# Loading q and k as two halves, and the order of Pool's work within a head, in an attention and MLP kernel

## The reference, cut to what matters

```python
batch, n_heads, seq, head_dim = (2, 8, 768, 64)
n_clusters = 16
...
q_assign = np.argmax(np.einsum('bhsd,hcd->bhsc', q_n, c_n), axis=-1)
k_assign = np.argmax(np.einsum('bhsd,hcd->bhsc', k_n, c_n), axis=-1)
mask = q_assign[:, :, :, None] == k_assign[:, :, None, :]
scores = scale * np.matmul(q, k.transpose(0, 1, 3, 2))
scores = np.where(mask, scores, -1000000000.0)
...
return np.matmul(attn, v).astype(np.float32)
```

## Time and profile before

| what | us |
| --- | --- |
| median of 3 runs | 767.41 |
| lowest and highest | 765.59, 771.37 |
| time of the profiled execution | 765.31 |
| its span, first to last instruction | 763.5 |

### The profile page before, as it was taken

How to read it: one execution, slowest core, us unless ns; L and a number is a source line. 1 busy time by engine, 2 the same in 40 slices (tenths; PEclk the granted TensorE clock), 3 DMA queues, 4 the chain that set the end, 5 groups by cost and what they waited for, 6 DMA issues and landing times.

```text
span 763.5 us, 10199 instructions
## 1 busy us (share of the span) xinstructions
PE 711.2 (93%) x3867; PEld 631.7 (83%) x3867; DVE 398.6 (52%) x698; ACT 290.7 (38%) x604; POOL 283.9 (37%) x304
## 2 busy tenths in 40 slices
PE   4899899799998979989999999999999989899998
PEld 4788899789898978977888888888888879888886
DVE  3678888588979866585211321113111169885310
ACT  2377677566767756121010210102101055443320
POOL 3456646666645663407870000000023224740000
PEclk9999999899999999999999999999999999999999
DMA  4434423342334420203330000001031231000011
GB/s 143 130 92 112 124 73 75 99 127 54 95 90 124 120 48 1 63 28 97 110 97 1 0 1 1 0 1 56 0 111 56 50 102 42 28 14 28 28 42 55
DMA packets 26865, 48.09 MB, mean 63 GB/s; under 512 B 4032, under 2 KB 11456, under 8 KB 26560
## 3 DMA queue, kind: packets, MB, share of 16 engines
q1 hardware_dynamic: 24368, 39.49, 18.3%
q0 software_dynamic: 2448, 7.95, 3.3%
HBM read 36.41 MB, written 3.15 MB: 52 GB/s over the span
## 4 chain that ended last, share of the span: by engine, by line
PE 67%; DVE 13%; POOL 8%; ACT 4%; issue 3%; DMA 3%; SPq 2%; POOLq 0%; ACTq 0%; DVEq 0%
PE ps L1236 19%; PE ps L1352 17%; PE ps L1428 9%; PE ps L1414 6%; PE ps L1163 4%; PE ps L1149 4%; PE ps L1106 3%; DVE pt_l L807 2%; DVE row_min L800 2%; PE ps L1137 2%; DMA raw_qk<-in_k 2%; DVE mask_n L841 2%; PE ps L1138 2%; SPq L361 1%; ACT pt_h L636 1%
## 5 line engine op out<-in xcount | busy, mean ns | idle before, releaser
L1001 DVE SCALAR_TENSOR_TENSOR hid_l<-ps,hid_h 128x512 fp32r<-128x512 f32 x48 | 33.1, 690 | 203.6 <-ACT hid_h L708 203.6
L807 DVE TENSOR_TENSOR pt_l<-ps,pt_h 128x384 fp32r<-128x384 f32 x192 | 101.2, 549 | 43.1 <-ACT pt_h L636 42.3
L708 ACT ACTIVATE hid_h<-ps 128x512 fp32r<-128x512 f32 x48 | 28.7, 598 | 227.0 <-PE ps L1236 227.0
L636 ACT ACTIVATE pt_h<-ps 128x384 fp32r<-128x384 f32 x192 | 84.7, 490 | 76.6 <-PE ps L1149 75.7
L1149 PE MATMUL ps<-cst,prob 128*128 128x128 f32 x576 | 85.4, 285 | 15.1 <-ACT prob L624 9.4
L800 DVE TENSOR_REDUCE row_min<-ps 128x1 f32<-128x768 f32 x96 | 90.1, 939 | 18.0 <-PE ps L1138 17.9
L624 ACT ACTIVATE prob<-ps,row_min 128x768 f32<-128x768 f32 x96 | 87.0, 907 | 8.2 <-DVE row_min L800 7.9
L1149 PEld LDWEIGHTS ps<-cst,prob 128*128 128x128 f32 x576 | 67.2, 147 | 26.9 <-ACT prob L624 18.7
L1137 PE MATMUL ps<-k,q 80*128 80x384 f32 x192 | 75.8, 395 | 8.8 <-issue 8.0
L1352 PE MATMUL ps<-w_h,hid_h 128*128 128x512 f32 x192 | 76.1, 396 | 1.4 <-DVE x L956 1.4
L1352 PE MATMUL ps<-w_h,hid_l 128*128 128x512 f32 x192 | 75.5, 393 | 0.0
(11 more groups left out here) (158 smaller groups left out, 1607.8 us busy)
## 6 DMA issues: line engine op xcount, KB each, us to landing
w_raw<-in_moe_w_ch SPq DMA_DIRECT2D x24, 256.0 KB, 2.6
raw_d<-in_q SPq DMA_DIRECT2D x8, 384.0 KB, 3.4
raw_d<-in_k SPq DMA_DIRECT2D x8, 384.0 KB, 4.6
raw_qk<-in_q SPq DMA_DIRECT2D x16, 192.0 KB, 3.2
raw_qk<-in_k SPq DMA_DIRECT2D x16, 192.0 KB, 3.4
raw_v<-in_v SPq DMA_DIRECT2D x16, 192.0 KB, 2.5
q<-q SPq DMA_DIRECT2D x16, 192.0 KB, 2.7
k<-k SPq DMA_DIRECT2D x16, 192.0 KB, 2.7
```

The lines of the kernel that those rows point to most:

```text
L636: nc.scalar.activation(pt_h[a][:, R * hf:R * hf + R, (t % R) * P:(t % R + 1) * P], ps[:, 4 + hf, 0:HALF].rearrange("p (j c) -> p j c", j=R ...
L807: nc.vector.tensor_tensor(pt_l[a][part], ps[:, 4 + hf, 0:HALF].rearrange("p (j c) -> p j c", j=R), as_f32(pt_h[a][part]), ALU.subtract).th ...
```

## The change

The load of raw q and that of raw k get semaphores of their own. SyncE issues the load of the next q as soon as q is split, ahead of the copy of k and of the mask rows; the load of k keeps its place. Pool's `scale_q` waits for q alone, and the high part of k for k. Pool's order within a head was: split q and k, scale the next q, split w1, split v, fold. It becomes: split q and k, fold, scale the next q, split w1, split v.

```diff
             def serve(i, s, loads=True):
...
                 sp.dma_start(as_f32(q2[s][0:D, :]), as_f32(q1[s][0:D, :])).then_inc(q2_copied[s], 16)
+                if loads:
+                    sp.wait_ge(q_split, n + 1)
+                    load_q(ahead, 1 - s)
                 sp.wait_ge(k_high, n + 1)
                 sp.dma_start(as_f32(k2[s][0:D, :]), as_f32(k1[s][D:2 * D, :])).then_inc(k2_copied[s], 16)
...
                 if loads:
-                    sp.wait_ge(q_split, n + 1)
                     sp.wait_ge(k_split, n + 1)
-                    load_qk(ahead, 1 - s)
+                    load_k(ahead, 1 - s)
...
             def scale_q(n):
 
-                pool.wait_ge(qk_loaded, 32 * n + 32)
+                pool.wait_ge(q_loaded, 16 * n + 16)
...
                 if n == 0:
                     return
+                pool.wait_ge(k_loaded, 16 * n + 16)
                 high(k1[s][D:P, :], raw_qk[D:P, :]).then_inc(k_high, 1)
...
             for n in range(1, NH):
                 split_qk(n, n % 2)
+                if n >= 5 and (n - 5) % 4 < 2:
+                    fold_block((n - 5) % 4, (n - 5) // 4)
                 if n < NH - 1:
                     scale_q(n + 1)
                 if n < W1_EARLY:
                     split_w1(n)
                 split_v(n, n % 2)
-                if n >= 5 and (n - 5) % 4 < 2:
-                    fold_block((n - 5) % 4, (n - 5) // 4)
```

More of the change, by code:

```diff
@@ L178, in build @@
         cst_loaded, cen_loaded = sem("cst_loaded"), sem("cen_loaded")
-        qk_loaded, v_loaded = sem("qk_loaded"), sem("v_loaded")
+        q_loaded, k_loaded, v_loaded = sem("q_loaded"), sem("k_loaded"), sem("v_loaded")
         q2_copied = [sem(f"q2_copied{s}") for s in range(2)]
@@ L337, in _, with load_q, load_k @@
             sp.dma_start(cen[:, 0, :], centroids.rearrange("h c d -> (h c) d")).then_inc(cen_loaded, 16)
-            def load_qk(i, s):
-                for j, t in enumerate((q_t, k_t)):
-                    sp.dma_start(raw_qk[j * D:(j + 1) * D, :], t[s, i, :, :]).then_inc(qk_loaded, 16)
+            def load_q(i, s):
+                sp.dma_start(raw_qk[0:D, :], q_t[s, i, :, :]).then_inc(q_loaded, 16)
+            def load_k(i, s):
+                sp.dma_start(raw_qk[D:2 * D, :], k_t[s, i, :, :]).then_inc(k_loaded, 16)
             def load_v(i, s):
@@ L385, in _ @@
             sp.dma_start(cst[:, :], constants).then_inc(cst_loaded, 16)
-            load_qk(0, 0)
+            load_q(0, 0)
+            load_k(0, 0)
             load_v(0, 0)
@@ L788, in _ @@
                 nc.vector.tensor_copy(cen_b[rows, :, par * C:(par + 1) * C], src).then_inc(cen_built, 1)
-            dve.wait_ge(qk_loaded, 32)
+            dve.wait_ge(k_loaded, 16)
             nc.vector.tensor_copy(k1[0][D:P, :], raw_qk[D:P, :]).then_inc(k_high, 1)
```

## The result

The changed kernel takes 757.22 us in the median of 4 runs (755.80 to 759.27), the kernel before 766.65 (4 runs): a ratio of 0.987, 95% interval 0.983 to 0.991, so 9.4 us less, against 756.0 and 11.4 forecast. Six later runs gave 758.40 against 765.81 for 11 runs of the kernel before: medians 7.4 us apart, ratio 0.988 (0.985 to 0.991). The profiled execution is the slowest of the first four: time 759.27, span 757.5.

The account below looks back on a forecast made before the run. TensorE's matmuls bound the kernel, with stalls where Pool was late with scores. Stalls -12.66, masks +2.7 and prologue +0.4 gave -9.6 from 765.31: 755.7, or 757.8 for the median; 756.0 was written, range 749 to 762.

Parts of the forecast that it names:

- The stalls: TensorE's waits before the first score matmuls of heads 7, 11 and 15, with slow clock: all go, -12.66 us.
- The signs for a late load: On Pool and TensorE: w1 making Pool wait more than 4.4 us after k's issue, or a score matmul still waiting.
- The masks: VectorE's six mask pairs meet Pool's q and k splits at a fixed phase: 13.8 us against 11.1, +2.7.
- the gate of v: Pool's split of v, 1.6 us, waits for the values of two heads back, is used much later, costs nothing.
- ports decide: Rival: VectorE's denominators too meet Pool in every head, +16.7 us, masks +6.2; slower, 775 us; chance 0.04.
- The prologue: Scaling of the early-loaded q of head 1 may meet the first mask pair: 0 to +0.8, taken as +0.4 us.
- The sum's own way to the median: 755.7 us for the profiled execution, with the median 2.1 above it, would give 757.8; 756.0 was written.
- The sign that showed: Prediction wrong if the heads' pace away from the stalls rises by more than the masks do; masks forecast +2.7 us.
- The sign against falls of the clock: TensorE's granted clock in the profile after should lack the two stretches of 0.50.
- Masks cheap: Rival: Pool's splits and VectorE's masks miss each other, up to -7.4 us more; 745 to 752, said 750; chance 0.20.
- A stall stays: Rival: k and w1 wait behind the mask store, or w1 lands late; half a large stall remains; 760 us; chance 0.14.
- The split of the credit: Pool's lap with a fold, halves and new order together: 15.3 us instead of 20.8.

Follow-up runs that it names:

- second profile: Profile from the later runs of the changed kernel, repeated with no edit: 758.40 us against 765.81 for the kernel before.
- experiment 7: The kernel of experiment 4 without the addition of 1e-9 to the denominators, the reciprocal reading the row sums: 744.27 us, 746.65 in a repetition.
- experiment 9: The kernel of experiment 7 with q of head 1 loaded in its old place, behind the mask rows: 744.17 us against 746.65 without this edit.
- experiment 4: The changed kernel with Pool waiting for VectorE's mask pair ahead of the q split in odd heads 3 to 13: 747.46 us.
- Experiments 2 and 3: First, the changed kernel with the fold back in its old place: 756.03 us. Second, the kernel before with the fold behind the split of k: 757.15 us.
- experiment 6: The kernel before with Pool's new order, the joint load kept, and Pool's wait for the mask pairs in odd heads 3 to 13: 747.84 us.

## Why the prediction was right

Right in direction, near in size (757.2 for 756.0, inside 749 to 762), and right in its two main steps, the stalls that go and the masks that grow. The nearness of the number is in part luck, and one sign that it had named for being wrong did show:

- *The stalls.* Forecast -12.66, measured -13.1: heads 6 and 14 to the expected 16.97 and 14.62, no clock fall there. The lead was at least as large as reckoned: q of head 6 was split 2.2 behind the mark ahead of it (111.68 - 109.47) where the forecast had 3.8 (110.7 - 106.92), and q of head 7 at 127.74, 0.25 behind a mark, with Pool waiting at its gate (126.0 forecast, 136.73 before). The signs for a late load did not show: w1 was used 3.6 to 4.4 us after k's issue, and no score matmul waited.
- *The masks.* Forecast 13.8 us of pairs, measured 14.0 and 13.8, at the phase named (q splits 0.25 to 0.56 behind a mark in heads 7 to 12). The gate behind that phase was another in most heads: the prediction had the split of q held by the scores of two heads back and said of the gate of v only that it costs nothing; in fact Pool was held at v, and q followed 1.57 behind the opening of that gate. That the two gates give the same phase within some 0.3 us is a coincidence of this kernel. But the forecast counted only the pair's own excess. The odd heads 1 to 11 took 98.05 before, 100.3 in the second profile (+2.3) and 103.2 in the first (+5.1), the difference being two falls of the clock behind the longest pairs. That such a wait can let the clock fall stood in the prediction only for the stalls, not for what takes their place.
- *Left out of the sum.* The denominators of heads 12 and 13, +1.5 together (15.58 twice for 14.78 and 14.87), and the hit weights of head 4, +1.05, which took 1.60 us (124.27) instead of 0.55 beside Pool's split of w1 (123.46 to 125.46); the denominators stood in the rival "ports decide", with slack as the argument against, the hit weights nowhere. Most denominators had slack, these had not (experiment 7). Head 2 gave 0.6 back.
- *The prologue.* Forecast +0.4; 1.2 in the first profile, and 1.6 by the means of all profiles (experiment 9). The term that was too small is the +0.4: it held the first mask pair alone (0.84 for 0.63 in the first profile), and not the work of head 1 that follows earlier and meets the second dots' masks (the hit weights at 1.70 for 0.94). TensorE's wait for these masks grew from 2.35 to 3.17.
- In the ledger of the first profile, -13.1 + 5.1 + 1.5 + 1.05 - 0.6 + 1.2 = -4.8 up to the mark of head 14; another 1.2 came behind it, where the kernel before had had a fall of the clock in the MLP. The span fell by 6.0, and the median by 9.4. The 3.4 between them are the choice of executions: the profiled one of the kernel before was 1.3 under its median, that of the changed kernel 2.0 over. In the second profile, without the two falls of the clock, it is -8.25 from the first mask pair to the mark of head 14, and -4.8 in the first, for the -9.6 forecast. So by execution the sum was 1.4 to 4.8 us too large, which the medians do not show. The sum's own way to the median, 757.8, was nearer than the 756.0 written.
- *The sign that showed.* The prediction was to be wrong "if the heads' pace away from the stalls rises by more than the masks do". It did: these heads took 7.1 us more in the first profile and 4.2 in the second, the pairs 2.9 and 2.7. The sign against falls of the clock failed in the first profile too, which has two new ones.
- *The rivals.* "Masks cheap" did not come by itself, but experiment 4 made it: 747.5, where the rival said 745 to 752. "A stall stays" did not happen; with the halves alone 0.4 and 0.9 us were left. "Ports decide" names the mechanism of what was left out, at a much smaller size.
- *The split of the credit.* The prediction gave the lap's new length to halves and order together. Experiments 2 and 3 show that either suffices, the halves alone but for about 1 us. That both were needed is an impression of its working that is wrong.

The rule cited from the Trainium skill ("SBUF — State Buffer", section "Who interferes with whom") is borne out: pairs of 0.61 alone and 2.08 with Pool, ending 0.2 us behind a Pool instruction, and 10.9 us of time for keeping them apart. As it is cited it speaks of VectorE instructions with two SBUF inputs; the denominators read one tile, and that they stretch too is shown by their rows alone.

## What to carry to other kernels

When an engine stops being late, ask what its new phase meets: here Pool moved from lagging to being held by TensorE's gates at a fixed distance from its marks, and its splits then met VectorE's masks in every other head. An engine with time to spare can be told to wait for the moment in which it would be in the way; one semaphore wait bought 10.9 us, the change itself 7 to 9. And such a cost is worth removing only after the lag is gone: the same wait in the kernel before brought nothing.

## What the runs showed of the hardware

- A small VectorE instruction that reads SBUF can take ten times its length beside Pool: a 128x3 addition took 1.71 us instead of 0.16, for the length of one Pool subtraction (1.83).
- The length of a wait of TensorE did not tell whether its clock fell behind it. A wait of 1.73 us was followed by half speed in one execution of the changed kernel; one of 1.72 us in another, and one of 1.75 us in the kernel before (95.36), were not. In experiment 6 half speed began at about 124.5, and the waits shortly ahead of it were of 0.74 (ending at 121.96) and 0.48 (ending at 124.31).
- The spread of a kernel is not explained by such waits alone. The ten runs of the changed kernel lie between 755.8 and 759.4, the three quickest at a mean granted clock of 1.000. But kernels whose profile has no wait of TensorE over 1 us in heads 1 to 15 spread as much (743.85 to 747.74 over five runs in experiment 7, 745.42 to 749.84 over six in experiment 6) or less (747.05 to 748.31 over six in experiment 4), and eight of the twelve profiles have a stretch at half speed behind the attention, between 596 and 664 us.
